# Tables 384 columns apart, constants at equal places, and another order of the work ahead of the first tile

## The reference

```python
def _attn_ref(x) -> np.ndarray:
    X = np.fft.fft(x, axis=1)
    X = np.fft.fft(X, axis=2)
    return X.real.astype(np.float32)
...
    h = x @ w_in
    r = np.maximum(h, 0.0)
    g = r * r
    return (g @ w_out).astype(np.float32)
...
    h = x @ w_in
    g = h * np.cos(h)
    return (g @ w_out).astype(np.float32)
```

## Time and profile before

| | us |
|---|---|
| median of 3 runs | 1893.19 |
| lowest, highest | 1892.76, 1893.51 |
| profiled execution | 1893.86 |
| its span in the profile | 1891.8 |
| TensorE busy, share of the span | 1876.9, 99% |
| VectorE, ScalarE | 1432.0 (76%), 1260.5 (67%) |
| granted TensorE clock, mean | 1.0 of full |

### The profile page before, as it was taken

How to read it: one execution, slowest core, us unless ns; L and a number is a source line. 1 busy time by engine, 2 the same in 40 slices (tenths; PEclk the granted TensorE clock), 3 DMA queues, 4 the chain that set the end, 5 groups by cost and what they waited for, 6 DMA issues and landing times.

```text
span 1891.8 us, 21334 instructions
## 1 busy us (share of the span) xinstructions
PE 1876.9 (99%) x8452; PEld 1580.3 (84%) x8452; DVE 1432.0 (76%) x1665; ACT 1260.5 (67%) x1320; POOL 0.2 (0%) x4
## 2 busy tenths in 40 slices
PE   7999999999999999999999999999999999999999
PEld 5888888888888888888888888888888888888887
DVE  8978877876876887777787688677777777777666
ACT  6967756765765766676676576576667667567655
POOL 0000000000000000000000000000000000000000
PEclk9999999999999999999999999999999999999999
DMA  7742112113112111100111311210000000000000
GB/s 281 254 134 87 64 38 97 40 37 123 56 53 93 64 64 67 57 6 10 46 39 37 113 56 53 84 40 6 11 23 6 12 23 6 1 22 1 1 12 22
DMA packets 37955, 105.82 MB, mean 56 GB/s; under 512 B 4312, under 2 KB 14808, under 8 KB 37600
## 3 DMA queue, kind: packets, MB, share of 16 engines
q1 hardware_dynamic: 35840, 90.53, 14.0%
q10 hardware_dynamic: 2016, 13.94, 2.1%
HBM read 85.91 MB, written 27.82 MB: 60 GB/s over the span
## 4 chain that ended last, share of the span: by engine, by line
PE 97%; DMA 1%; DVE 1%; ACT 1%; issue 0%; SPq 0%; ACTq 0%
PE ps L969 96%; DMA stage_a<-w2i 1%; PE ps L987 0%; DMA wst<-w1i 0%; DVE gh L887 0%; DMA ab<-scratch_a 0%; DMA scratch_a<-est 0%; PE ps L992 0%; DVE kbuf L922 0%; DVE u L927 0%; DVE u L928 0%; ACT gh L702 0%; ACT u L696 0%; ACT u L703 0%; PE ps L1120 0%
## 5 line engine op out<-in xcount | busy, mean ns | idle before, releaser
L969 PE MATMUL ps<-gh,wo 128*128 128x502 f32 x4596 | 1089.0, 386 | 0.6 <-DVE gh L887 0.6
L969 PEld LDWEIGHTS ps<-gh,wo 128*128 128x128 f32 x4596 | 861.6, 188 | 166.9 <-DVE gh L887 2.8
L969 PE MATMUL ps<-y,wi 128*128 128x502 f32 x2304 | 545.3, 385 | 0.0
L969 PEld LDWEIGHTS ps<-y,wi 128*128 128x128 f32 x2304 | 431.9, 188 | 80.5
L934 DVE TENSOR_TENSOR u<-kbuf,ps 128x1004 f32<-128x1004 int32 x192 | 230.5, 1200 | 323.4 <-ACT kbuf L711 323.3
L887 DVE TENSOR_TENSOR gh<-u,gh 128x1004 fp32r<-128x1004 f32 x384 | 460.3, 1199 | 4.2 <-ACT u L703 2.1
L711 ACT ACTIVATE kbuf<-ps 128x1004 int32<-128x1004 f32 x192 | 193.8, 1010 | 326.9 <-PE ps L969 326.9
L696 ACT ACTIVATE u<-u 128x1004 f32<-128x1004 f32 x192 | 200.8, 1046 | 144.7 <-DVE u L928 143.6
L969 PE MATMUL ps<-eo,weo 128*128 128x502 f32 x1146 | 287.0, 385 | 0.0
L969 PEld LDWEIGHTS ps<-eo,weo 128*128 128x128 f32 x1146 | 215.0, 188 | 41.2 <-issue 0.2
L723 ACT ACTIVATE u<-u 128x1004 f32<-128x1004 f32 x192 | 200.5, 1045 | 65.0 <-DVE u L934 65.0
(11 more groups left out here) (93 smaller groups left out, 332.1 us busy)
## 6 DMA issues: line engine op xcount, KB each, us to landing
ring<-scratch_t SPq DMA_DIRECT2D x72, 378.0 KB, 4.0
xin<-x SPq DMA_DIRECT2D x36, 512.0 KB, 3.4
out<-io SPq DMA_DIRECT2D x23, 502.0 KB, 3.3
scratch_t<-tables ACTq DMA_DIRECT2D x12, 756.0 KB, 4.6
io<-scratch_eo SPq DMA_DIRECT2D x11, 502.0 KB, 5.1
scratch_eo<-est SPq DMA_DIRECT2D x14, 376.5 KB
stage_t<-tables SPq DMA_DIRECT2D x6, 756.0 KB, 16.9
tab_odd<-scratch_t ACTq DMA_DIRECT2D x2, 2268.0 KB, 11.8
```

What stands on the lines that cost most here:

```text
L969: op = pe.matmul(out_, a, b, start=start and i == 0, stop=stop and i == len(todo) - 1)
```

## The change

Tables: the 378 columns of each table part now stand 384 apart, in SBUF, in the DRAM copies and in the ring. Constants: `cs` is one row of 1032 columns, low parts at 0, high parts at 512 (before, the parts were 520 columns apart). `w128_product` reads its 512 columns in order, and ScalarE reorders them as it copies the result. The `fold` buffer shrinks, the second step of a fold works in place in `xin`, and so the next load of `xin` waits for step three of four (`folded`), not two (`paired`).

Start: nine matmuls on zeros first; `cin` and the first weights are loaded ahead of x; weight work goes ahead of the folds on ScalarE and VectorE; all `w128_product` calls but the last move up; VectorE copies table 5, not 4; tile 0's second half is made in two pieces; `ab` comes from one matmul with ones and a copy; `w1_high(3)` and `w1_low(3)` move behind tile 0's making and behind item 0's first VectorE work; the low part of item 0 is made in two halves, with a signal for each.

```diff
+KS = 384
...
-VECTOR_TABLE = 4
+VECTOR_TABLE = 5
+WARM_UP = 9
...
+    xin, fold, ring = area(A_F + 12288, A_F + 26624, ("xin", [P, 4, 2, P], F32), ("fold", [P, 2, P], F32),
+                           ("ring", [P, 3, 2, KS], F32R))
...
+    tab_even, = area(A_WI2, A_WI2 + 36864, ("tab_even", [P, 2 * KT, 2, 2, KS], F32R))
+    tab_odd, = area(A_WI2 + 36864, A_Y1 + 8192, ("tab_odd", [P, 2 * KT, 2, 2, KS], F32R))
...
-        A_GH, A_GH + 13312, ("wsp1", [P, 2, 2, WP], F32R), ("cs", [P, 2, 4 * P + 2 * WQ], F32R), ("lx", [P, 2 * KT, 4, B], F32),
+        A_GH, A_GH + 13312, ("wsp1", [P, 2, 2, WP], F32R), ("cs", [P, 8 * P + 2 * WQ], F32R), ("lx", [P, 2 * KT, 4, B], F32),
...
-            if t:
-                sp.wait_ge(u_done, last_of["up", t - 1, 0] + 1)
+            sp.wait_ge(u_done, last_of["up", t - 1, 0] + 1)
-                sp.wait_ge(paired, n)
+                sp.wait_ge(folded, n)
...
             sp.dma_start(out[sign, t].rearrange("h p k -> p h k"), osb[:, :, :]).then_inc(stored, 16)
         sp.dma_start(lx[:, :, :, :], x128).then_inc(lx_in, 16)
+        sp.dma_start(cin[:, :], consts).then_inc(c_in, 16)
+        load_w1(0)
         sp.dma_start(x0[:, 0, 0, :, :, :], x[0, 0, 0]).then_inc(x0_half_in, 16)
         sp.dma_start(x0[:, 0, 1, :, :, :], x[0, 0, 1]).then_inc(x0_in[0], 16)
-        sp.dma_start(cin[:, :], consts).then_inc(c_in, 16)
-        load_w1(0)
         load_w1(1)
         load_x0(1)
         load_w1(2)
...
         for n in range(2 * KT):
             load_even_table(n)
         load_w1(3)
-        for n in range(4):
+        load_split(0)
+        load_w128(0)
+        for n in range(1, 4):
             load_split(n)
-        load_w128(0)
+        load_w128(1)
         store_rows(0)
-        sp.wait_ge(est_st, 16)
-        load_a(0)
         sp.wait_ge(rows_out, EARLY)
         sp.dma_start(scratch_eo[0, :, :, 0:KP].rearrange("e p k -> p e k"), est0[:, :, 0:KP]).then_inc(est0_st, 16)
-        load_w128(1)
         load_split(4)
...
-            act.activation(wrow[i][0:WQ, :], w128ps, ACT.Copy).then_inc(row_out, 1)
+            act.activation(wrow[i][0:WQ, :].rearrange("q (k i) -> q k i", i=WQ), w128ps.rearrange("q (i k) -> q k i", k=P),
+                           ACT.Copy).then_inc(row_out, 1)
...
-        act.activation(cs[:, 0, :], cin[:, :], ACT.Copy).then_inc(c_hi, 1)
-        even_high(0)
+        act.activation(cs[:, 4 * P:], cin[:, :], ACT.Copy).then_inc(c_hi, 1)
         w1_high(0)
         w1_high(1)
-        even_high(1)
+        even_high(0)
+        copy_w128(0)
         weo_high(0)
         w1_high(2)
-        copy_w128(0)
+        even_high(1)
+        weo_high(1)
         table_parts(0)
-        weo_high(1)
+        copy_w128(1)
         table_parts(1)
+        weo_high(2)
+        table_parts(2)
         even_high(2)
-        table_parts(2)
-        weo_high(2)
         table_parts(3)
         copy_odd_rows(0)
+        table_parts(4)
         copy_odd_rows(1)
-        table_parts(5)
+        act.wait_ge(odd0, 2)
+        act.wait_ge(tile_rows, 1)
+        act.activation(eo[0][:, 0, :], est0[:, 0, 0:T], ACT.Copy).then_inc(eo_hi, 1)
+        n = columns_of(0)[0]
+        act.wait_ge(rows_done, 3)
+        act.activation(est0[:, 1, n:n + TH], early[2][:, 1, 0:TH], ACT.Copy).then_inc(part_copied, 1)
+        act.activation(est0[:, 1, n + TH:2 * n], early[2][:, 1, TH:n], ACT.Copy).then_inc(odd_copied, 1)
+        act.wait_ge(part_rows, 1)
+        act.activation(eo[0][:, 1, 0:TH], est0[:, 1, 0:TH], ACT.Copy).then_inc(part_hi, 1)
+        act.wait_ge(tile_rows, 2)
+        act.activation(eo[0][:, 1, TH:T], est0[:, 1, TH:T], ACT.Copy).then_inc(eo_hi, 1)
+        act.wait_ge(a_sum, 1)
+        act.activation(ab[:, :], ps[1][:, 0, 0:T], ACT.Copy).then_inc(a_made, 1)
         w1_high(3)
-        copy_odd_rows(2)
-        act.wait_ge(odd0, 2)
-        for phase in range(2):
-            act.wait_ge(tile_rows, phase + 1)
-            act.activation(eo[0][:, phase, :], est0[:, phase, 0:T], ACT.Copy).then_inc(eo_hi, 1)
-        copy_w128(1)
...
+        dve.memset(zeros[:, :].bitcast(F32), 0.0).then_inc(zeros_set, 1)
+        dve.memset(ones[0:1, :], 1.0).then_inc(ones_set, 1)
...
         dve.wait_ge(last_hi, 1)
         dve.tensor_tensor(lastc[1][:, 0:4 * KT * B], lfold[:, :, :, :].rearrange("p e t b -> p (e t b)"),
                           lastc[0][:, 0:4 * KT * B].bitcast(F32), ALU.subtract).then_inc(last_lo, 1)
+        dve.wait_ge(c_hi, 1)
+        dve.tensor_tensor(cs[:, 0:4 * P], cin[:, 0:4 * P], cs[:, 4 * P:8 * P].bitcast(F32), ALU.subtract).then_inc(c_lo, 1)
+        w1_low(0)
         fold_first(0)
-        dve.wait_ge(c_hi, 1)
-        dve.tensor_tensor(cs[:, 1, :], cin[:, :], cs[:, 0, :].bitcast(F32), ALU.subtract).then_inc(c_lo, 1)
+        w1_low(1)
         even_low(0)
-        w1_low(0)
-        w1_low(1)
         fold_first(1)
+        w1_low(2)
         even_low(1)
-        fold_first(2)
-        w1_low(2)
         dve.wait_ge(wsp_lo, 3)
         weo_low(0)
+        fold_first(2)
         weo_low(1)
+        fold_odd(0)
         even_low(2)
-        fold_odd()
+        fold_odd(1)
         weo_low(2)
+        take_rows(0)
         dve.wait_ge(t_in[VECTOR_TABLE], 16)
-        dve.tensor_copy(tab_even[:, VECTOR_TABLE, :, :, :], stage_t[:, VECTOR_TABLE, :, :, :]).then_inc(te_hi_dve, 1)
-        take_rows(0)
+        dve.tensor_copy(tab_even[:, VECTOR_TABLE, :, :, 0:KH], stage_t[:, VECTOR_TABLE, :, :, 0:KH]).then_inc(te_hi_dve, 1)
         take_rows(1)
         finish_rows(1)
-        w1_last_low(0)
-        take_rows(2)
-        for phase in range(2):
-            dve.wait_ge(eo_hi, phase + 1)
-            dve.tensor_tensor(eo[1][:, phase, :], est0[:, phase, 0:T], eo[0][:, phase, :].bitcast(F32),
-                              ALU.subtract).then_inc(eo_lo, 1)
+        def tile_low_part(phase, first, last):
+            return dve.tensor_tensor(eo[1][:, phase, first:last], est0[:, phase, first:last],
+                                     eo[0][:, phase, first:last].bitcast(F32), ALU.subtract)
+        dve.wait_ge(eo_hi, 1)
+        tile_low_part(0, 0, T).then_inc(eo_lo, 1)
+        n = columns_of(0)[0]
+        dve.wait_ge(part_copied, 1)
+        dve.tensor_tensor(est0[:, 1, 0:TH], early[2][:, 0, 0:TH], est0[:, 1, n:n + TH], ALU.add).then_inc(part_rows, 1)
+        dve.wait_ge(odd_copied, 3)
+        dve.tensor_tensor(est0[:, 1, TH:n], early[2][:, 0, TH:n], est0[:, 1, n + TH:2 * n],
+                          ALU.add).then_inc(plus_done, 1)
+        dve.wait_ge(part_rows, 1)
+        dve.wait_ge(plus_done, 3)
+        subtract_rows(2, 0, T - n).then_inc(tile_rows, 1)
+        dve.wait_ge(part_hi, 1)
+        tile_low_part(1, 0, TH)
+        dve.wait_ge(eo_hi, 2)
+        tile_low_part(1, TH, T).then_inc(eo_lo, 1)
         finish_rows(2)
...
-                if n:
-                    dve.wait_ge(fold_lo, n)
-                dve.tensor_tensor(fold[:, 1:3, :], xin[:, 0:2, 0, :], xin[:, 0:2, 1, :],
+                dve.tensor_tensor(xin[:, 0:2, 0, :], xin[:, 0:2, 0, :], xin[:, 0:2, 1, :],
-                dve.tensor_tensor(fold[:, 0, :], fold[:, 1, :], fold[:, 2, :], ALU.add)
-                dve.tensor_tensor(fold[:, 1, :], fold[:, 1, :], fold[:, 2, :], ALU.subtract).then_inc(folded, 1)
+                if n:
+                    dve.wait_ge(fold_lo, n)
+                dve.tensor_tensor(fold[:, 0, :], xin[:, 0, 0, :], xin[:, 1, 0, :], ALU.add)
+                dve.tensor_tensor(fold[:, 1, :], xin[:, 0, 0, :], xin[:, 1, 0, :], ALU.subtract).then_inc(folded, 1)
+            if it.c == 0:
+                for sign, done in enumerate((plus_lo, g_lo)):
+                    dve.tensor_tensor(gh[1][:, place, sign, :], u[:, place, sign, :],
+                                      gh[0][:, place, sign, :].bitcast(F32), ALU.subtract).then_inc(done, 1)
+                return
...
-                if it.index == 0:
-                    dve.wait_ge(a_in, 16 * (it.t + 1))
+                if it.index == 0 and it.t == 0:
+                    dve.wait_ge(a_made, 1)
+                elif it.index == 0:
+                    dve.wait_ge(a_in, 16 * it.t)
-                if it.c == 1:
+                if it.c == 0:
+                    w1_low(3)
...
-                return cs[:, part, (2 * e + kt) * P:(2 * e + kt + 1) * P]
+                return cs[:, (4 * (1 - part) + 2 * e + kt) * P:][:, 0:P]
+                pe.wait_ge(a_made, 1)
...
-            at_ = 4 * P + WQ - 1 - q
+            at_ = 8 * P + WQ - 1 - q
-                    op = pe.matmul(w128ps, cs[:, 0, at_:at_ + WQ], wsp[q][half][:, kt, :].rearrange("p (i k) -> p k i", k=P),
+                    op = pe.matmul(w128ps, cs[:, at_:at_ + WQ], wsp[q][half][:, kt, :],
-                op = row_step(r, kt, parity, lambda i: tab[odd][:, KT * phase + kt, parity, i, :])
+                op = row_step(r, kt, parity, lambda i: tab[odd][:, KT * phase + kt, parity, i, 0:KH])
+        pe.wait_ge(zeros_set, 1)
+        for _ in range(WARM_UP):
```

(39 more changed lines are left out.)

39 lines of the change are left out of this document (17 added, 22 removed).

## The result

| | before | after |
|---|---|---|
| median, us | 1893.01 (6 runs) | 1969.45 (6 runs) |
| lowest, highest | 1892.45, 1893.51 | 1968.96, 1969.88 |
| profiled execution, its span | 1893.86, 1891.8 | 1968.96, 1967.0 |
| ratio, 95% interval | | 1.0404 [1.039, 1.0417] |

A forecast was written before the change was run, and what follows sets the result against it. After 92 us only the number of TensorE matmuls and the time of one were taken to count. Start -1.6, `tab_odd` load +0.2 and tables -0.8 made -2.2 us: from 1893.2 to 1891.0, range 1888.2 to 1893.4.

The forecast's parts named there:

- The new start: Start up to tile 0: item 0 on VectorE at 34.2 for 36.03 us, 1.6 us of gain going on to tile 0.
- The anchor: Loads of the even tables: landing times left as before, the first at 19.25 us and the last at 28.5.
- rival 5: Start: loads land sooner as x's large rows come later, and VectorE keeps up; 1.5 us more, 1889.5 us; chance 0.07.
- Rival 3: Start: gives nothing, since VectorE was full from 20 us on and its work is only reordered; 1892.6 us; chance 0.12.
- The load of `tab_odd`: Tile 0: a load waits behind the two `tab_odd` loads (11.8 us), which grow by 1.6%; 0.2 us lost.
- rival 6: Folds: `xin` released later, so an x landing over 7.6 us stops VectorE, up to 1903 us; chance 0.03.
- a fall of the clock: Before the tile: thinner TensorE work lets the clock fall to 1.2 GHz, costing 6 us, 1897 us; chance 0.02.
- The slow side: Whole kernel slower by over 0.2%, through a late x landing or a clock fall; chance 0.05.
- The tables: Row products: parts 384 apart make 270 matmuls of 378 columns 3 ns shorter each, 0.8 us gained.
- The last line of the forecast: Long matmuls: if they change, the new places' effect on them was missed, 1 ns being 8 us in all.
- rival 2: Row products: the places of the tables do nothing and the walk of the start holds; 1891.8 us; chance 0.15.
- rival 4: Row products: the tables save all that is over, 4.4 us instead of 0.8; 1887.4 us; chance 0.06.

## Why the prediction was wrong, step by step

**The new start: right, somewhat under.** TensorE's and VectorE's timeline of after:

```profile
1.44 3.90 PE L1073 MATMUL ps<-zeros 128*128 128x512 f32 x9 [1.44 <-DVE zeros L829]
...
6.63 2.09 PE L1022 MATMUL ps<-wsp,cs 128*128 128x512 f32 x8 [1.28 <-ACT wsp L524]
...
9.47 1.07 PE L1035 MATMUL ps<-wsp,cs 128*4 128x512 f32 x4
...
27.91 0.93 DVE L861 CAST tab_even<-stage_t 128x1512 fp32r<-128x1512 f32 x1
...
30.13 1.10 PE L1099 MATMUL ps<-est,ones 1*128 1x502 f32 x2
...
40.09 1.51 PE L1003 MATMUL ps<-gh,wo 128*128 128x502 f32 x6
...
44.80 2.95 PE L1003 MATMUL ps<-gh,wo 128*128 128x502 f32 x12
```

| step | before | foretold | after |
|---|---|---|---|
| first product of TensorE | 10.90 | 6 to 8 | 6.63 |
| copy of table 0 | 19.3 | 19.3 | 18.26 |
| VectorE's copy of table 5 | | 29.0 | 27.91 |
| item 0 on VectorE | 36.03 | 34.2 | 33.57 |
| `down` of item 0 | 42.51 | 40.5 | 40.09 |
| `down` of item 1 | 46.91 | 45.3 | 44.80 |

The copy of table 5 was indeed late by VectorE and not by its load, `down` of item 0 did run in two halves around `weo_low(3)` (40.09 and 41.83), and the gain did fall from 2.4 to 2.1 us on the way to item 1. The anchor was off: table 0 landed 13.0 us after its issue for 14.0, at 18.2, and the last at 27.7 (8.4 and 19.3) for 28.5. Of that microsecond 0.6 was left at item 0, where rival 5 had 1.5. Rival 3, that the front gives nothing, falls: at the handover 1.6 us are left. The matmul with ones took 1.10 us in two records, not 0.22, and was hidden as assumed. The nine matmuls on zeros took 3.90 us, and the first eight products then 2.09 for 3.78: the zeros started 427 ns apart and the products 227 to 232, so the clock came up to its upper level on the zeros, though the column of the granted clock shows 1.00 for both. The products with four columns took 1.07 for 1.13, hidden as assumed. But the medians keep less of it than the traces show: 1892.07 for 1892.94 with the best kernel, 0.9 us, where its 8088 matmuls begin 2.2 us sooner (89.80 for 92.02). The two profiled executions lie at opposite ends of their runs (1891.58 is the lowest of eight, 1893.86 above every other of before on that occasion), and the interval takes in no change: the gain stands in the traces and isn't clear of noise in the times.

**The load of `tab_odd`: right in itself.** 12.0 us for 11.8. The load behind it took 10.89 for 10.38, so 0.5 was lost there where the sum had 0.2, and the gain at the handover came out at 1.6 for 1.4.

**The next x, rival 6: nothing of it.** Landings of `xin` in after, against the earlier trace rows:

```profile
DMA to landing us min/median/max: 3.1/3.3/5.0
```

Its other half, a fall of the clock, didn't come either: the first six matmuls of 378 columns took 1.27 us and the next twelve 2.25, so they ran at the upper level. The slow side was named, and priced at 4 to 10 us, for mechanisms that had no part in it.

**The tables: here it failed.** The step is "The 502 columns stand 512 apart and start at equal places; the 378 do not ... If only this differs, a short one comes down by 2 ns". Three things were wrong in it. The size: 1.4 ns for 3, so 0.3 us in the 216 of the ring for the 0.8 of all 270; the 54 from `tab_odd` took 9.9 us in both kernels. The reason: 380 apart, unequal places, saves more than 384. And above all the figure 223.4 for a long matmul was taken as the property of that instruction, from a mean over 7818 of them, and the sum left them out because their operands didn't change. They were one of two paces, and in after the pace was set by how the stream left row product 4, with the parts 384 apart: 233.3 ns on 7752 matmuls, 77.5 us that the sum had at nothing. The row for it stood in the trace of before: 24 matmuls in 5.75 us at 102 us, where 24 at 223.4 make 5.52. Comparing two stretches with the same operands would have shown it. The last line of the forecast had the price right, 1 ns for 8 us, and gave it no chance. None of the rivals had the long matmuls changing: rival 2 (nothing from the places, 1891.8) was nearest to what they do to the short ones, and rival 4 (4.4 us) falls.

The Trainium skill ("TensorE: Matmul & The Clock Gate", Part 2, on the gap of back-to-back issue) gives an isolated warm matmul N/2.4 and 2.5 ns, which for 502 columns makes an estimate of 211.7, and says that in a stream of weight loads and matmuls both together set the spacing. The trace has neither 211.7 nor one value, but 223.3 or 233.3; that the weight loads have a part in it is what the late load at 1393.79 suggests, and no run here shows it.

## What stays open

What the two paces are inside TensorE, and why they are 223 and 233. Why row product 4 from `tab_odd` at 384 ends in 233 while ring products at 384 keep 223: they differ in the weight operand (`lastc` for `fa`) and in number (18 for 9), and this wasn't taken apart; nor was row product 3, which goes the other way round. Why the late load of each tile changes the pace in some executions and not in others, and on some occasions and not on others: a load 58 ns late did it once, and four others of 58 ns, in three traces, didn't. Whether pauses, which remove these late loads, guard against it on an occasion with spread.

The best of these kernels has the new start, `tab_odd` and `tab_even` at 378 and the ring at 384: 1892.07 beside 1892.94, an interval that takes in 1. Keeping the new start rests on the 1.6 to 2.2 us of the traces; `tab_odd` at 384 is what must not be kept.

## What to carry to other kernels

A duration per instruction from a stream that is never interrupted is the stream's, not the instruction's: compare its spacing in several stretches before a sum leaves it out, for 10 ns on 7750 matmuls is 77 us, where the whole new start gave two. When a kernel that is bound by TensorE moves by per cents after an edit elsewhere, count matmuls in equal windows first, and find the first window in which they differ. A short wait at that place is a cheap experiment, and it tells a state from a cost. When executions of one kernel are spread, see whether their lengths come in steps, and which place in the loop the steps point at.

## What the runs showed of the hardware

- Loads of weights and matmuls of 502 columns in turn run at 223.3 or 233.3 ns from start to start, with the same operands and the granted clock at 1.00 in both; either lasts for more than 1700 us. Matmuls of 378 columns show no such difference.
- Row products of 378 columns whose parts stand 378 or 380 apart in the ring ended in 223; 384 apart they kept the pace they found, either of the two. From `tab_odd` the stream came out at 233, 223 and 223 behind row products 3, 4 and 5 at 378, and at 223, 233 and 233 at 384.
- Once in each tile but the last a weight load came 48 to 59 ns behind the matmul ahead of it, 52 to 55 ns behind the end of the VectorE instruction that it waited for. Two such loads, of 58 and 59 ns, stand where a stream went from 223 to 233; others of up to 58 ns changed nothing.
- With a pause of 0.32 us behind row product 5, none of 11 executions had the length of after on one occasion (highest 1914.59), and 4 of 10 came near it on another (1967.3 to 1968.65).
- The parts' distance changes a matmul of 378 columns by up to 3.2 ns: 41.6, 40.9 and 41.3 us for 216 of them at 378, 380 and 384.
- A matmul of plain float32 with one row of weights and 502 columns has two records and takes 1.10 us.
